# Attention and two MLPs on one core: q and k loads of the third pair moved ahead of v and of the first weights, and all key sums added on GpSimd

## What is computed

```python
batch, n_heads, seq, head_dim = (2, 12, 448, 64)       # q, k, v; cap = 30
n_tokens, d_model, d_ff = (896, 768, 2048)             # both MLPs

scores = cap * np.tanh((q @ k.T) / sqrt(64) / cap)
attn = np.exp(scores - scores.max(-1))
attn = attn / (attn.sum(-1) + 1e-9)
x = (attn @ v), heads side by side, reshaped to (896, 768)
x = square(relu(x @ w_in1)) @ w_out1
x = silu(x @ w_in2) @ w_out2
```

## Time and profile before

| what | value |
|---|---|
| time, median of 3 runs | 586.72 us (586.72 to 586.93) |
| the profiled execution's own time | 586.58 us |
| its span, first to last instruction | 584.8 us |
| attention, until the first MLP matmul | 0 to 108.65 us |
| the two MLPs and the stores | 108.65 to 584.8 us |
| mean granted TensorE clock | 0.993 |

### The profile page before, as it was taken

One profiled execution on the slowest core, in us unless ns is written; L12 is line 12 of the kernel. 1 busy time (PEld: TensorE's weight loads), 2 busy tenths in 40 slices (PEclk: granted clock), 3 DMA queues, 4 the chain that ended last, 5 costly groups with the idle time before them and its releaser, 6 DMA issues.

```text
span 584.8 us, 7972 instructions
## 1 busy us (share of the span) xinstructions
PE 565.7 (97%) x2800; PEld 466.0 (80%) x2800; DVE 223.1 (38%) x403; ACT 167.4 (29%) x207; POOL 54.3 (9%) x42
## 2 busy tenths in 40 slices
PE   5599999999999999999999999999999999999996
PEld 3133333499999999999999999999999999999996
DVE  2177977975555555121202123333333302120210
ACT  4578888422222222021202113222222201010100
POOL 1535655400000000000000000000000000000000
PEclk9989999999999999999999999999999999999999
DMA  5745544211111122212121102111112221212553
GB/s 141 188 106 155 146 129 123 67 34 56 54 54 54 55 62 67 69 39 69 41 66 40 49 28 67 56 53 55 54 54 62 62 66 47 62 46 63 92 86 48
DMA packets 83122, 41.93 MB, mean 72 GB/s; under 512 B 27808, under 2 KB 80032, under 8 KB 83104
## 3 DMA queue, kind: packets, MB, share of 16 engines
q1 hardware_dynamic: 81952, 41.13, 26.4%
q10 hardware_dynamic: 1120, 0.57, 0.5%
q0 software_dynamic: 32, 0.00, 0.0%
HBM read 38.93 MB, written 2.75 MB: 71 GB/s over the span
## 4 chain that ended last, share of the span: by engine, by line
PE 90%; SPq 4%; DMA 2%; DVE 2%; issue 1%; DVEq 0%
PE ring L371 13%; PE o_t L371 13%; PE o_t L373 13%; PE ring L373 13%; PE ring L372 13%; PE o_t L372 13%; PE o_t L324 4%; PE ring L312 3%; SPq L190 2%; DMA qk_raw<-in_q_dram 1%; PE o_t L333 1%; PE ring L309 1%; PE o_t L322 1%; SPq L206 1%; DMA qk_raw<-in_k_dram 1%
## 5 line engine op out<-in xcount | busy, mean ns | idle before, releaser
L689 DVE TENSOR_TENSOR w_lo<-w_raw,w_hi 128x768 fp32r<-128x768 f32 (+1 forms) x56 | 60.0, 1072 | 292.6 <-ACT w_hi L495 292.6
L495 ACT ACTIVATE w_hi<-w_raw 128x768 fp32r<-128x768 f32 (+1 forms) x56 | 52.5, 938 | 358.8 <-PE ring L373 182.8
L371 PE MATMUL ring<-x_hi,w_hi 128*128 128x448 f32 x384 | 140.4, 366 | 0.0
L371 PE MATMUL o_t<-g_hi,w_hi 128*128 128x448 f32 x384 | 140.2, 365 | 0.0
L373 PE MATMUL o_t<-g_hi,w_lo 128*128 128x448 f32 x384 | 140.2, 365 | 0.0
L372 PE MATMUL ring<-x_lo,w_hi 128*128 128x448 f32 x384 | 140.2, 365 | 0.0
L372 PE MATMUL o_t<-g_lo,w_hi 128*128 128x448 f32 x384 | 140.2, 365 | 0.0
L373 PE MATMUL ring<-x_hi,w_lo 128*128 128x448 f32 x384 | 140.2, 365 | 0.0
L371 PEld LDWEIGHTS ring<-x_hi,w_hi 128*128 128x128 f32 x384 | 72.1, 188 | 7.2 <-issue 1.5
L372 PEld LDWEIGHTS o_t<-g_lo,w_hi 128*128 128x128 f32 x384 | 72.1, 188 | 5.7
L371 PEld LDWEIGHTS o_t<-g_hi,w_hi 128*128 128x128 f32 x384 | 72.1, 188 | 5.7
(11 more groups left out here) (44 smaller groups left out, 249.9 us busy)
## 6 DMA issues: line engine op xcount, KB each, us to landing
w_raw<-in_moe_w_in_dram SPq DMA_DIRECT2D x32, 384.0 KB, 3.4
w_raw<-in_moe_w_out_dram SPq DMA_DIRECT2D x24, 512.0 KB, 3.9
qk_raw<-in_k_dram SPq DMA_DIRECT2D x48, 112.0 KB, 2.4
qk_raw<-in_q_dram SPq DMA_DIRECT2D x44, 112.0 KB, 2.5
out_dram<-rows SPq DMA_DIRECT2D x46, 56.0 KB, 2.2
v_t<-in_v_dram SPq DMA_DIRECT2D x48, 48.0 KB, 1.8
v_x<-in_v_dram SPq DMA_DIRECT2D x48, 8.0 KB, 1.6
qk_raw<-in_q_dram ACTq DMA_DIRECT2D x4, 112.0 KB, 4.3
```

The costliest lines, as they stand in the source:

```text
L371: pe.matmul(dst, w_hi[par][:, kk, :], mov_hi, start=start, stop=False)
L495: act.activation(w_hi[n.par][:, 0:blocks, :], w_raw[n.par][:, 0:blocks, :], ACT.Copy).then_inc(s_w_hi, 1)
L689: dve.tensor_tensor(w_lo[n.par][:, 0:blocks, :], w_raw[n.par][:, 0:blocks, :], w_hi[n.par][:, 0:blocks, :].bitcast(F32), ALU.subtract).the ...
```

## The change

Four things change.

1. SP: v of pair 1 is loaded after q and k of pair 2, and the two weight loads move from ahead of q and k of pair 2 to behind `load_pair` of pair 10, ahead of v of pair 11. ACT makes both high parts between pairs 10 and 11 (before: one behind pair 1, one between 10 and 11). DVE makes the low parts around `finish(9)`.
2. POOL adds unit 2 as well, in one more instruction of 128x896 between the two that were there, so `sums` has two matmuls with 64 columns of ones in place of four with 32.
3. DVE: `finish` loses the four copies across 32 rows, and its add is a plain tensor_scalar.
4. ACT: for pair 0 all four tanh come ahead of the two exps.

```diff
@@ -69,7 +69,7 @@
         qk_scale = sb(ctx, "qk_scale", [P, 1])
         eps_e = sb(ctx, "eps_e", [P, 1])
         eps_t = sb(ctx, "eps_t", [P, 1])
-        o_sel = sb(ctx, "o_sel", [P, BL])
+        ones = sb(ctx, "ones", [P, D])
         w_raw = [sb(ctx, f"w_raw{i}", [P, WK, P]) for i in range(2)]
         w_hi = [sb(ctx, f"w_hi{i}", [P, WK, P], F32R) for i in range(2)]
         w_lo = [sb(ctx, f"w_lo{i}", [P, WK, P], F32R) for i in range(2)]
@@ -93,7 +93,6 @@
             colmax = sb(att, "colmax", [P, 2, S])
             rowmax = sb(att, "rowmax", [P, 2, S])
             den_r = sb(att, "den_r", [P, S])
-            den_x = sb(att, "den_x", [P, QB])
             den = sb(att, "den", [P, QB])
             rinv = sb(att, "rinv", [P, S])
             att_o = sb(att, "att_o", [P, S])
@@ -221,12 +220,10 @@
             load_part(At(0, 0), 0, k_v, s_first_in[0])
             sp.wait_ge(s_first_in[0], 4 * DMA)
             load_qk(At(0, 1))
-            for j in range(2):
-                load_v(At(0, j))
-            for f in range(2):
-                load_w_in(0, At(0, f), At(0, f))
+            load_v(At(0, 0))
             sp.wait_ge(s_turned, 2)
             load_qk(At(0, 2))
+            load_v(At(0, 1))
 
             def load_pair(j):
 
@@ -237,6 +234,8 @@
 
             two_steps(sp, 2, PAIRS - 4, load_pair)
             load_pair(At(0, PAIRS - 2))
+            for f in range(2):
+                load_w_in(0, At(0, f), At(0, f))
             sp.wait_ge(s_att, PAIRS - 2)
             load_v(At(0, PAIRS - 1))
 
@@ -274,11 +273,13 @@
                 t, a = prob[j.par], asum[j.par]
                 pool.tensor_tensor(a[:, :, :], t[:, 0:2, :], t[:, 2:4, :], ALU.add).then_inc(s_sum, 1)
                 pool.wait_ge(s_exp, 2 * j.no + 2)
+                pool.wait_ge(s_sum, 4 * j.no + 1)
+                pool.tensor_tensor(a[:, :, :], a[:, :, :], t[:, 4:6, :], ALU.add).then_inc(s_sum, 1)
                 for h in range(2):
                     rp = slice(D * h, D * h + D)
-                    pool.wait_ge(s_sum, 3 * j.no + 1 + h)
+                    pool.wait_ge(s_sum, 4 * j.no + 2 + h)
                     pool.tensor_tensor(a[rp, h, :], a[rp, h, :], t[rp, 2 * CW, :], ALU.add).then_inc(s_sum, 1)
-                pool.wait_ge(s_sum, 3 * j.no + 3)
+                pool.wait_ge(s_sum, 4 * j.no + 4)
 
             with pool.If(shifted(pool)):
 
@@ -326,11 +327,9 @@
 
             def sums(j):
 
-                pe.wait_ge(s_sum, 3 * j.no + 3)
-                for g in range(4):
-                    h = g // 2
-                    mov = asum[j.par][:, h, :] if g % 2 == 0 else prob[j.par][:, 4 + h, :]
-                    last = pe.matmul(o_t[j.par][BL * g:BL * g + BL, 1, 0:S], o_sel[:, :], mov,
+                pe.wait_ge(s_sum, 4 * j.no + 4)
+                for h in range(2):
+                    last = pe.matmul(o_t[j.par][D * h:D * h + D, 1, 0:S], ones[:, :], asum[j.par][:, h, :],
                                      start=True, stop=True)
                 last.then_inc(s_att, 1)
 
@@ -496,12 +495,21 @@
                                ACT.Copy).then_inc(s_w_hi, 1)
 
             act.wait_ge(s_scale, 4)
-            for j in range(2):
-                weights(At(0, j))
-            weight_high(At(0, 0), KC)
+            for u in range(C):
+                tanh(At(0, 0), u)
+            with act.If(off_max):
+                act.wait_ge(s_shift, 5)
+                exp(At(0, 0), 0)
+                exp(At(0, 0), 1)
+            with act.Else():
+                act.wait_ge(s_ring, C)
+                exp(At(0, 0), 0)
+                exp(At(0, 0), 1)
+            weights(At(0, 1))
             two_steps(act, 2, PAIRS - 4, weights)
             weights(At(0, PAIRS - 2))
-            weight_high(At(0, 1), KC)
+            for f in range(2):
+                weight_high(At(0, f), KC)
             weights(At(0, PAIRS - 1))
 
             def hidden_act(layer, f):
@@ -562,7 +570,7 @@
 
         @block.vector
         def _(dve):
-            dve.memset(o_sel[:, :], 1.0).then_inc(s_fill, 1)
+            dve.memset(ones[:, :], 1.0).then_inc(s_fill, 1)
             dve.memset(eps_t[:, :], EPS).then_inc(s_eps_t, 1)
             dve.wait_ge(s_cap, DMA)
             dve.tensor_scalar(cap_n[:, :], cap_b[:, :], -1.0, None, ALU.mult).then_inc(s_scale, 1)
@@ -596,20 +604,15 @@
 
                 dve.wait_ge(s_att, j.no + 1)
                 dve.transpose(den_r[:, :], o_t[j.par][:, 1, 0:S]).then_inc(s_den, 1)
-                dve.wait_ge(s_den, 8 * j.no + 1)
-                part = den_r[:, :].rearrange("p (b i) -> p b i", i=BL)[:, :, 0]
-                for g in range(4):
-                    o = g + 1 - 2 * (g % 2)
-                    dve.tensor_copy(den_x[BL * g:BL * g + BL, :], part[BL * o:BL * o + BL, :]).then_inc(s_den, 1)
-                dve.wait_ge(s_den, 8 * j.no + 5)
-                dve.scalar_tensor_tensor(den[:, :], part, eps_t[:, 0:1], den_x[:, :],
-                                         op0=ALU.add, op1=ALU.add).then_inc(s_den, 1)
-                dve.wait_ge(s_den, 8 * j.no + 6)
+                dve.wait_ge(s_den, 4 * j.no + 1)
+                dve.tensor_scalar(den[:, :], den_r[:, :].rearrange("p (b i) -> p b i", i=BL)[:, :, 0],
+                                  eps_t[:, 0:1], None, ALU.add).then_inc(s_den, 1)
+                dve.wait_ge(s_den, 4 * j.no + 2)
                 dve.reciprocal(den[:, :], den[:, :]).then_inc(s_den, 1)
-                dve.wait_ge(s_den, 8 * j.no + 7)
+                dve.wait_ge(s_den, 4 * j.no + 3)
                 dve.transpose(rinv[:, :].rearrange("p (b i) -> p b i", i=BL),
                               den[:, :].unsqueeze(2).to_broadcast([P, QB, BL])).then_inc(s_den, 1)
-                dve.wait_ge(s_den, 8 * j.no + 8)
+                dve.wait_ge(s_den, 4 * j.no + 4)
                 dve.tensor_tensor(att_o[:, :], o_t[j.par][:, 0, 0:S], rinv[:, :], ALU.mult).then_inc(s_norm, 1)
                 dve.wait_ge(s_norm, j.no + 1)
                 dve.tensor_copy(x_hi[:, bass.ds(j.no, 1), :], att_o[:, :].unsqueeze(1)).then_inc(s_x_hi, 1)
@@ -706,12 +709,13 @@
             shift(At(0, 0))
             prepare(At(0, 2))
             shift(At(0, 1))
-            weight_low(At(0, 0), KC)
             two_steps(dve, 2, PAIRS - 4, slot)
             slot(At(0, PAIRS - 2))
             shift(At(0, PAIRS - 1))
+            weight_low(At(0, 0), KC)
+            finish(At(0, PAIRS - 3))
             weight_low(At(0, 1), KC)
-            for j in range(PAIRS - 3, PAIRS):
+            for j in range(PAIRS - 2, PAIRS):
                 finish(At(0, j))
 
             for layer in range(2):
```

## The result

| what | before | changed |
|---|---|---|
| time, median (lowest to highest) | 586.72 us (586.52 to 586.93) | **589.55 us** (589.32 to 590.75) |
| ratio of the medians, 95% interval | | **1.0056 (1.0041 to 1.007)** |
| profiled execution, time / span | 586.58 / 584.8 us | 590.75 / 588.8 us |
| mean granted clock | 0.993 | 0.996 |
| scores of pair 2 start | 28.68 us | 26.66 us |

A forecast was written before the change was run, and what follows sets the result against it. SP's issue, 8.12 us a pair, was taken to pace the attention's middle. Scores (unit 2) of pair 11 3.0 us earlier, after 2.9 given back, plus sums twice 0.14, made 3.3: 586.58 to 583.3, predicted 583.4, range 580.0 to 587.0.

The forecast's parts named there:

- Middle: SP's loop over pairs: eight periods of 8.12 us bring q and k of pair 11 to 87.3, 5.0 us earlier.
- the 1.3 us that the prediction had named and set aside: SP's loop: one long v_x issue group, 3.19 us instead of about 1.85, expected not to recur; otherwise all 1.3 us later.
- Start: Start of attention: reordered loads, then first sums waiting for POOL, put pair 2's scores at 23.6 instead of 28.68, 5.1 earlier.
- the stall at the weights: End of attention: ACT waits at w_hi for late weights, delaying pair 11's scores (unit 2); 2.9 us given back.
- Rival b): End of attention: the 2.9 us TensorE stall lets the clock fall, costing 2.5 us, 585.9 us; chance 0.12.
- two matmuls of the rest unit: Sums on TensorE: two 64-column matmuls take 0.75 us like the rest unit's, instead of 0.89, saving 0.14 a slot.
- The change leaves that part as it is: The two MLPs: their chain is TensorE alone and was expected to stay unchanged.
- rival d: Middle: POOL's three back-to-back instructions hold DVE; 589.1 us, chance 0.10, or no change at about 586.6, chance 0.04.
- the two waits at the end: End of attention: ACT idle 3 us ahead of w_hi near 95 us, and TensorE idle ahead of scores (unit 2).
- Rival a): End of attention: no stall because weights land sooner or SP runs ahead; 2.9 us more gain, 580.5 us; chance 0.12.
- Rival c): Middle: transfers, not issues, are the limit, so TensorE's 7.53 us a slot sets the pace; 576.8 us; chance 0.04.
- Rival e): Start: first sums wait for POOL, so pair 2 comes no earlier; needs POOL 5 us later; no chance of its own.

The follow-up runs named there:

- e11_tiles_where_they_were: Changed, with ones in the attention's region and an unused 32-column tile in o_sel's place, so the weight tiles lie as in before: 587.61 us.
- e4_tanh_as_before: Changed, with pair 0's tanh and exp on ACT back in the old order: 590.69 us.
- g1_changed_warm16: Changed, with the weight tiles where they lay in before and 16 warm-up matmuls instead of 8: 586.78 us.
- e12_and_weights_at_start: Changed, with the weight tiles where they lay in before and the two weight loads moved behind v of pair 1: 584.83 us.
- e2_no_shift: Changed, with ones moved to the attention's region and nothing in its place, weight tiles 128 bytes lower than in before: 589.47 us.
- e1_shift_only: Before, with an unused 32-column tile behind o_sel, so all weight tiles lie 128 bytes higher: 588.22 us.
- e9_front_alone: Before, with q and k of pair 2 loaded ahead of v of pair 1 and the two weight loads behind both: 585.23 us.
- e10_front_unrolled: Before, with q and k of pair 2 ahead of v of pair 1, weight loads behind both, and SP's pair loop written out: 584.37 us.
- e3_w_pair_earlier: Changed, with the two weight loads one load_pair earlier, ahead of q and k of pair 11: 589.24 us.
- g3_middle_and_warm16: Before, with SP's new front, loop written out, weights loaded behind pairs 5 and 7, w_hi around pair 10, and 16 warm-up matmuls: 583.93 us.
- e6_sums_part_alone: Before, with only the new sums (unit 2 added on GpSimd, two matmuls, finish without copies), weight tiles unmoved: 587.10 us.
- g2_weights_in_middle: Before, with SP's new front, loop written out, weights loaded behind pairs 5 and 7, and w_hi around pair 10: 582.04 us.

## Why the prediction was wrong

The span was put at 581.5 us and came to 588.8. The 7.3 us between are four terms:

- **+3.15, the start and the first turn of SP.** S, the issue of q and k of pair 11, was put at 87.3 and was 90.45. Of this 0.12 is there at SP's loop entry (22.47 for 22.35), 2.79 in the first turn (10.91 for 8.12), the rest in the second. The step that failed is in "Middle". There v of pair 2 waits for sums(0) "at 23.5, long past", and of the long group of issues the prediction says "I take it to belong to the crowded transfers and not to come again". The sums ended at 26.7, which cost 0.6, and long groups came in the first turn with no weights in flight, which cost most of the rest. In three kernels of this kind in which SP did not wait for the sums the first turn still took 9.25 to 9.43 us (e11_tiles_where_they_were, e4_tanh_as_before, g1_changed_warm16): this is the 1.3 us that the prediction had named and set aside. Before it, in "Start", "The second exp ends at about 17.4" was built on the one trace of before, in which the first scores ran at full pace. g1_changed_warm16 gives that step back when the pace is full, but its S is 89.08 all the same.
- **+0.29, the stall at the weights.** Scores (unit 2) came at S + 15.14 for S + 14.85, values of pair 10 at S + 9.47 for S + 9.5. This chain was right. Its price of 2.9 is near the 3.20 us that TensorE stood idle. That the medians of e11_tiles_where_they_were and e12_and_weights_at_start differ by 2.8 is no proof of it: that difference holds lost clock and a later S too, and at full clock the two traces differ by 1.9 from S on. Since S had moved by 1.85 instead of 5.0, the stall was larger than the gain that it was set against.
- **+2.0, from there to the first MLP matmul, and the last sums.** 1.7 is the clock. Rival b) was this, at a chance of 0.12, on the ground that the rows showed the loss only behind 6.7 us idle. It came behind 3.20. The profiles of e2_no_shift, e4_tanh_as_before and g1_changed_warm16, with 2.46, 2.89 and 2.92 us idle at this place, keep 1.00. The other 0.28 is the sums, twice 0.14: they took 0.90, not 0.75. The nearest row, two matmuls of the rest unit, was the wrong one. It multiplies 64 rows and not 128; that this is what makes it shorter is not shown.
- **+1.8, the MLPs.** "The change leaves that part as it is" failed. The diff's first hunk moved the tiles of the weights by 128 bytes, and the matmuls on x pay for it: 1.6 us by e1_shift_only, 1.5 in the trace of e11_tiles_where_they_were. Neither the sum, nor a bound, nor a rival had a place for it.

Right were SP's 8.12 us a pair as the pace of the middle once the start is early, no cost of the busier POOL in the middle (rival d did not come: DVE's prepare starts 5.8 to 6.0 us behind SP's issue in each pair), a clock of 1.0 from 20 to 40 us, and the two waits at the end with their places. Rival a) did not come. Rival c) had a point of its own: with the loop written out the issues go at 7.45 us a pair where SP waits for nothing, so 0.67 of the 8.12 comes with the loop and its register addresses, not with the transfers. Rival e) held in part, as of the 5.1 us 2.0 were left at pair 2, with 1.04 of waiting for POOL.

In medians: the front of SP with the weights at the start gains 1.4 us (e9_front_alone), the weights moved from there to the end cost 2.8, the placement 1.6, the sums nothing that can be told. That gives a loss of about 3, and 2.8 was measured. The new order of tanh was tested only against changed, and showed nothing in the median.

**What stays open.** What decides whether the clock falls. In the profiles it fell behind idle pieces of 2.51 us (e10_front_unrolled), 2.66 (e3_w_pair_earlier), 3.05 (e11_tiles_where_they_were), 3.16 (g3_middle_and_warm16) and 3.20 (changed), and held behind 2.46, 2.89 and 2.92, so the length of the piece alone does not sort them. Why before started at full pace in one profile. What holds one issue of SP for over a microsecond in its first turns. Why 128 bytes matter: that it is the distance between the weights' tiles and those of x is the likeliest reading, since g moved with the weights and cost nothing, but no run moved x. And 0.3 us of the MLPs: kernels with the new sums, e6_sums_part_alone too, have it with steps of 7.30.

## What to carry to other kernels

A tile that grows moves all tiles allocated behind it. Where one phase takes 80% of the time, compare its step in the two traces before anything else, and pad the old place when the edit is meant for another phase. A load moved off a busy start must go where the queue has slack and several microseconds before its reader: at the end of the attention the weights cost 2.8 us more than at its start, and in the middle nobody waited for them. And time gained at the start is real only if the next loads keep up; a gain that ends in an idle piece of 2.5 to 3 us can lose the clock with it.

## What the runs showed of the hardware

- With the tiles of the weights 128 bytes higher or lower, x in place, a step of 36 matmuls of 128x448 took 7.34 us instead of 7.30, 0.5% more.
- The first scores, 2.4 to 2.9 us behind the end of the warm-up, ran partly or wholly at half pace in fourteen of fifteen profiles (up to 3.36 us for 1.77; before, with 2.44 us idle, kept 1.77). Six of the fourteen show a granted clock of 0.50 there, the other eight read 1.00 and took 3.35 or 3.36 us. With a warm-up of twice the matmuls, which ended 0.2 to 1.0 us before the scores, they took 1.77 in three kernels; whether its length or its end does it was not told apart.
- Ahead of pair 11's scores (unit 2), TensorE idle for 3.05 and 3.20 us was followed by a clock of 0.50 (e11_tiles_where_they_were, changed), idle for 2.46 to 2.92 by 1.00 in three kernels. Elsewhere the clock fell behind 2.51 and 2.66 us too.
- DVE's small tensor_scalar of 128x14 took 0.23 us alone and up to 1.73 beside an add on GpSimd, as x_hi did in the earlier trace rows. Without den_x the hold moved to the next instruction.
- Sixteen issues of 8 to 112 KB went at 7.45 us written out with constant addresses (g2_weights_in_middle) and at 8.12 in a loop with register addresses.
